# Two routed mixture layers on one core: the last scatters of the convolution phase and the first block weights at other places in the program

## The chip, the cores and the metric

The kernel runs on one NeuronCore of a Trainium2 chip. What counts is the device time of one execution in microseconds (us). PE is the matrix engine (TensorE), DVE VectorE, ACT ScalarE, POOL GpSimd and SP SyncE, which here issues transfers alone. Sixteen DMA engines carry every transfer, whichever queue issues it.

## The reference

`x` has 4 x 3584 tokens of 192 numbers. A causal convolution with 7 taps comes first (one softmaxed kernel for each of 8 groups of 24 columns), then two top-1 mixture layers over its 14336 rows. Cut to what matters:

```
x   = conv(x, softmax(weight))                  # 14336 rows of 192
for layer in (0, 1):
    logits = x @ w_gate                         # 8 experts
    e      = argmax(logits, 1)
    gate   = softmax(logits)[e]                 # in layer 1 also * sigmoid(x @ w_output_gate)[e]
    x[i]   = gate[i] * (relu(x[i] @ w1[e]) @ w2[e])     # w1 192x1024, w2 1024x192
```

## The kernel before

**The convolution phase** has 8 steps of 16 windows of 112 rows. In a step PE convolves, transposes the rows and computes the gate's logits; DVE picks the expert of each row (`step_choose`), and PE's `ranks` and DVE's `step_place` give each row its place in a buffer sorted by expert (`rows[0]` in HBM). POOL then writes the step's rows there with 16 indirect DMAs of 112 rows each (`scatter_step`): 8 of them, then the maximum of the next step's weights, then the other 8. In step 7 no weights follow, so the second half of step 6's scatters stands right behind its first half, and the 16 of step 7 come as soon as their indices are there (`index_ready`).

**The tiles.** Each layer then has 60 tiles, numbered 0 to 59 and 60 to 119, four to a quad. A tile is 256 sorted rows of one expert. PE multiplies them with w1 in four chunks (`hidden`), each of which raises `h_done`; ACT makes the high half of the hidden values when it sees `h_done` (L797, `hh`), DVE the low half (L1352, `hl`), and PE multiplies both with w2 (`contract`): chunk 0 of a tile at the end of that tile, chunks 1 to 3 between the next tile's. ACT writes the result to `y` (L809). From quad 4 of each layer on every third tile of a quad is made of two blocks of 128 rows with an expert each; their weights lie in two slots of their own, slot 2 (the memory of `split`) and slot 3 (the memory of `stage`).

**Who sets the order.** Every engine runs a program of its own, written out by hand. SP's is `loads`: at tile g it waits for `h_done` of tile g, issues the first part (w1, 1 MB) of the weights for tile g+1 if the expert changes, the transposes that bring the rows of tile g+2, and after `y_done` the second part (w2, 0.75 MB). Four tiles of a layer, those with `first`, also load slots 2 and 3, a part each. POOL in layer 0's tiles fetches, scales and stores the next layer's weights and scatters the rows of layer 0's results, four indirect DMAs for two tiles (L626), each held back by `paced` until PE has reached a given chunk. `EARLY` says how many tiles of each layer are planned from a part of the counts: the first 14 tiles of layer 0 use rows of steps 0 to 5 alone. Which expert a tile has stands in a table that DVE writes (`tab` row 0); `tab` row 2 holds the change of expert against two tiles before, since even and odd tiles use slots 0 and 1 in turn. `blk` is the table for blocks, done with `table_ready` 3.

Of the kernel before, what the change touches and what calls it, by code (L numbers as in the profile page):

```python
# [20 lines left out]
E, F = 8, 1024  # L21
N = B * S
P = 128
# [8 lines left out]
G = 16  # L32
STEPS = WINS // G
SPB = STEPS // B
# [11 lines left out]
NT = WHOLE + MIXED  # L46
GT = 2 * NT
EARLY = (14, 12)
QUADS = NT // 4
MIXQ = QUADS - MIXED  # L50
# [24 lines left out]
def build(nc, x, weight, wg0, w10, w20, wg1, wo1, w11, w21, out):  # L75
    f32, f16, i32 = mybir.dt.float32, mybir.dt.float16, mybir.dt.int32
# [11 lines left out]
    with ctx:  # L88
        def sb(name, shape, dt):
            return ctx.enter_context(nc.sbuf_tensor(name, shape, dt))  # L90

        def sem(name):
            return ctx.enter_context(nc.semaphore(name))
# [73 lines left out]
        took = sb("took", [P, E], f32)  # L167
        offr = sb("offr", [P, E + 1], f32)
        start = sb("start", [P, 1], f32)
        ge = sb("ge", [P, NT, E], f32)  # L170
        gt = sb("gt", [P, NT, E], f32)
        te = sb("te", [P, NT], f32)
        tst = sb("tst", [P, NT], f32)
        tew = sb("tew", [P, NT], f32)
        tabD = sb("tabD", [P, GT], f32)
        tab = sb("tab", [P, 3, GT], i32)
# [67 lines left out]
        table_ready = sem("table_ready")  # L244
# [18 lines left out]
        def late(t, n):  # L263

            return not isinstance(t, int) or t >= n
# [9 lines left out]
        def quad(body, i, prep, l, mix):  # L275

            for c in range(4):
                body(i * 4 + c, i * 2 + c // 2, c % 2, c // 2, i, prep, l, mix)

        def layer_of(g, l):  # L280

            return int(g >= NT) if isinstance(g, int) else l
# [46 lines left out]
                 ((QUADS + 2, QUADS + MIXQ, False, False), (QUADS + MIXQ, 2 * QUADS - 1, False, True)))  # L329
        TAIL = range(GT - 4, GT)  # L330
        LAST = (GT - 1, (GT - 1) // 2, 1)
        assert NT % 4 == 0 and 1 < MIXQ < E + 1 < QUADS - 1 and max(EARLY) <= 4 * MIXQ and 12 <= min(EARLY) and STEPS == E and SPB == 2

        def steps(eng, body):

# [38 lines left out]
        def _(sp):  # L374
# [24 lines left out]
            for n in range(STEPS):  # L399
                other = (n + 1) % 2  # L400
# [23 lines left out]
            def load_x(g, x, l):  # L424
                load_rows(tab[0:1, 1, bass.ds(g, 1)], 0, T, x, l, x_loaded[x], meta_loaded[x])
# [5 lines left out]
            def expert(g):  # L431
                return sp.value_load(tab[0:1, 0, bass.ds(g, 1)], min_val=0, max_val=E - 1)

            def block_expert(i, a):
                return sp.value_load(blk[0:1, 0, a, bass.ds(i, 1)], min_val=0, max_val=E - 1)

            def load_w_part(e, l, slot, part):
                cols = (slice(0, W2H), slice(W2H, WCOL))[part]
                sp.dma_start(wslots[slot][:, cols], images[l][bass.ds(e + l, 1), :, cols].rearrange("e p c -> (e p) c")).then_inc(w_loaded[part][slot], 16)

            def change(g):
                return sp.value_load(tab[0:1, 2, bass.ds(g, 1)], min_val=1 - E, max_val=E - 1)
# [13 lines left out]
            def loads(g, k, s, v, i, prep, l, mix):  # L456

                last = g if isinstance(g, int) else 0
                other = isinstance(g, int) and g + 1 in (EARLY[0], EARLY[0] + 1, NT, NT + 1, NT + EARLY[1], NT + EARLY[1] + 1)
                c, ahead = 2 * v + s, layer_of(g + 1, l)  # L460
                first = isinstance(g, int) and i % QUADS == MIXQ - 1
                again = mix and c == 3 and not (isinstance(g, int) and i % QUADS == QUADS - 1)
                needs = []
                if late(g, 1):
                    sp.wait_ge(h_done, g * NP)
                    sp.sem_inc(store_turn, 1)
                    if last + 1 < GT and not (mix and c == 1):
                        needs.append((None if other else change(g + 1), lambda: expert(g + 1), ahead, 1 - s))
                for need in needs:
                    load_next(*need, 0)  # L470
                if last + 2 < GT:
                    if late(g, 1):
                        sp.wait_ge(meta_out, g)
                    if mix and c == 0:
                        load_blocks(i, 2, l)
                    else:
                        load_x(g + 2, (c + 2) % XS, layer_of(g + 2, l))
                if first:
                    load_w_part(block_expert(i + 1, v), l, 2 + v, s)
                for a in range(2 if again else 0):  # L480
                    needs.append((block_change(i + 1, a), lambda a=a: block_expert(i + 1, a), l, 2 + a))
                    load_next(*needs[-1], 0)
                if needs:
                    sp.wait_ge(y_done, g)
                    sp.sem_inc(store_turn, 1)
                for need in needs:
                    load_next(*need, 1)
# [6 lines left out]
            first = [expert(g) for g in range(2)]  # L494
# [9 lines left out]
            for g in HEAD:  # L504
                one(loads, g)
            with sp.Fori(1, 2) as i:
                quad(loads, i, False, 0, False)
            sp.wait_ge(pads_ready, 1)
            for c in range(E // 2):
                one(loads, 8 + c)  # L510
                for e in (2 * c, 2 * c + 1):
                    store_pad(sp, 0, e)
            sp.wait_ge(table_ready, 3)
            for i in range(2 * SLOTS):
                sp.wait_ge(scat_a[i], 8 * G * len(range(i // 2, STEPS, SLOTS)))
            for g in range(12, 4 * MIXQ):
# [19 lines left out]
            sp.wait_ge(table_ready, 5)  # L536
            for v in range(2):
                sp.wait_ge(scat_p[v], 16 * W2T * (PAIRS // 2))
            with sp.Fori(QUADS + 2, QUADS + MIXQ - 1) as i:
                quad(loads, i, False, 1, False)  # L540
            sp.wait_ge(table_ready, 6)
            for g in range(NT + 4 * MIXQ - 4, NT + 4 * MIXQ):
                one(loads, g)
            sp.wait_ge(pads_stored, 32 * E)
            with sp.Fori(QUADS + MIXQ, 2 * QUADS - 1) as i:
# [6 lines left out]
        def _(pool):  # L552
# [37 lines left out]
            def step(n, b, q):  # L590
                if late(n, 1):
                    scatter_step(n - 1, 0, G // 2)
                if n + 1 < STEPS:
                    weight_maxima(n + 1, 1 - q)
                if late(n, 1):
                    scatter_step(n - 1, G // 2, G)

            def weight_maxima(j, slot):
# [4 lines left out]
            def scatter_step(n, w0, w1):  # L603
                if w0 == 0:
                    pool.wait_ge(index_ready, n + 1)
                    pool.sem_inc(pool_turn, 1)
                for w in range(w0, w1):
                    nc.gpsimd.indirect_dma_start(  # L608
                        rows[0][:, :], bass.IndirectOffsetOnAxis(idxa[0:WIN, n % SLOTS, w:w + 1], 0),
                        rowa[n % SLOTS][0:WIN, w, :], None, bounds_check=ROWS - 1,  # L610
                        oob_is_err=False).then_inc(scat_a[2 * (n % SLOTS) + w // (G // 2)], 16)

            weight_maxima(0, 0)
            steps(pool, step)
            scatter_step(STEPS - 1, 0, G)
            def paced(chunk):
                pool.wait_ge(h_done, chunk)
                pool.sem_inc(pool_turn, 1)

            def scatter_row(p, v, j):  # L620
                if j == 0:
# [433 lines left out]
        def _(dve):  # L1055
            V = nc.vector
# [236 lines left out]
            def table_tiles(l, g0, n, unit, first, whole):  # L1293

                at_ = tidx[:, g0:g0 + n] if unit == T else bidx[:, 0:n]
                b3 = lambda a: a.unsqueeze(2).broadcast_to((P, n, E))
                e3 = lambda a: a.unsqueeze(1).broadcast_to((P, n, E))
                link(V.tensor_tensor(ge[:, 0:n, :], b3(at_), e3(cum[:, :]), ALU.is_ge))
                link(V.tensor_tensor(gt[:, 0:n, :], ge[:, 0:n, :], e3(til[:, :]), ALU.mult))
                V.tensor_reduce(tst[:, 0:n], gt[:, 0:n, :], AX.X, ALU.add)  # L1300
                link(V.tensor_reduce(te[:, 0:n], ge[:, 0:n, :], AX.X, ALU.add))
                link(V.scalar_tensor_tensor(tst[:, 0:n], at_, float(unit), tst[:, 0:n], ALU.mult, ALU.add))
                row = row_of(l, g0, n, unit)
                if first:
                    V.tensor_scalar(row, entries(tst, n, unit), float(CAP * E), None, ALU.min)
                else:
                    V.tensor_scalar(row, entries(tst, n, unit), start[:, 0:1], float(CAP * E), ALU.add, ALU.min)
                link(V.tensor_scalar(tew[:, 0:n], te[:, 0:n], float(E - 1), None, ALU.min))
                if unit == T:
                    V.tensor_tensor(tab[:, 2, g0 + 2:g0 + n], tew[:, 2:n], tew[:, 0:n - 2], ALU.subtract)  # L1310
                else:
                    te2 = entries(tew, n, unit)
                    V.tensor_tensor(blk[:, 2, :, g0 + 1:g0 + MIXED], te2[:, :, 1:MIXED], te2[:, :, 0:MIXED - 1], ALU.subtract)
                V.tensor_copy(expert_of(l, g0, n, unit), entries(tew, n, unit)).then_inc(table_ready, 1)
# [221 lines left out]
```

## Time and profile before

| | |
|---|---|
| median of 3 runs | 1329.62 us (1328.49 to 1333.94) |
| the profiled execution | 1330.72 us |
| its span, first to last instruction | 1329.2 us |
| PE busy | 1175.1 us, 88% of the span |
| DVE / ACT / POOL busy | 855.4 / 615.7 / 438.4 us |
| mean granted PE clock | 0.926 of full |

The profile has the start, length and engine of each instruction, and for each wait the engine or DMA that ended it. Where no instruction's end explains the update that ended a wait, the row says "remote"; where an engine waited for nothing that the profile shows, it says "issue". The convolution phase takes the first 250 us or so, the tiles the rest.

### The profile page before, as it was taken

How to read it: one execution, taken by the hardware profiler on the slowest of the kernel's cores; microseconds unless marked ns; L12 is line 12 of the kernel's file. 1: busy time of each engine (PE TensorE's matmuls, PEld its weight loads, DVE VectorE, ACT ScalarE, POOL GpSimd, SP SyncE). 2: the span in 40 equal slices, each digit the busy share in tenths (PEclk: the TensorE clock that was granted, in tenths of full speed). 3: DMA queues.
4: the chain of work that ended last, by engine and by line, in shares of the span. 5: the costliest groups of instructions: out<-in, count | busy, mean ns of one | idle time of the engine just before them, and what ended most of it. 6: DMA issues, size and time to landing. Idle time of an engine off the chain costs nothing.

```text
span 1329.2 us, 38842 instructions
## 1 busy us (share of the span) xinstructions
PE 1175.1 (88%) x13470; PEld 1063.7 (80%) x13470; DVE 855.4 (64%) x2331; ACT 615.7 (46%) x1083; POOL 438.4 (33%) x478
## 2 busy tenths in 40 slices
PE   3767565379998999999999999999999999999996
PEld 2666564358886888888999989788899998999996
DVE  3888778448996998998777787654333433434332
ACT  2766666125554555555555444333333333333332
POOL 1277767522432433333222222322222222222222
PEclk9676765679998999999999999999999999999998
DMA  8677864728979789856544446338824545424451
GB/s 253 193 228 252 255 212 141 210 46 207 231 219 313 144 232 293 231 156 192 140 105 103 106 104 160 64 105 197 247 58 111 163 114 162 114 53 105 113 135 52
DMA packets 236335, 216.61 MB, mean 163 GB/s; under 512 B 176927, under 2 KB 209339, under 8 KB 230114
## 3 DMA queue, kind: packets, MB, share of 16 engines
q1 hardware_dynamic: 209696, 150.68, 43.3%
q0 software_dynamic: 25520, 64.49, 16.2%
q8 instruction: 41, 0.67, 0.2%
q10 hardware_dynamic: 1042, 0.47, 0.2%
q14 instruction: 36, 0.29, 0.1%
HBM read 116.05 MB, written 69.62 MB: 140 GB/s over the span
## 4 chain that ended last, share of the span: by engine, by line
PE 60%; DVE 19%; issue 8%; DMA 4%; another core or an unknown queue 3%; ACT 3%; SPq 2%; DVEq 0%; POOL 0%; ACTq 0%; POOLq 0%
PE bank L856 59%; DMA wslot<-image 2%; DVE am L1120 2%; DVE hl L1352 2%; DVE split L1195 1%; PE bank L861 1%; DVE wam L1084 1%; DVE split L1198 1%; ACT rowt L713 1%; DVE wslot L1222 1%; DVE rowab L1129 1%; DVE rowt L1129 1%; DMA stage<-in_moe_w 1%; DVE wam L1082 1%
## 5 line engine op out<-in xcount | busy, mean ns | idle before, releaser
L1352 DVE SCALAR_TENSOR_TENSOR hl<-bank,hh 128x512 f16<-128x512 f32 x480 | 331.1, 690 | 360.8 <-ACT hh L797 319.3
L797 ACT ACTIVATE hh<-bank 128x512 f16<-128x512 f32 x480 | 286.2, 597 | 487.7 <-PE bank L856 403.5
L856 PE MATMUL bank<-xT,wslot 128*128 128x256 f16 (+1 forms) x3920 | 468.0, 275 | 15.1 <-issue 7.2
L856 PE MATMUL bank<-wslot,hh 128*128 128x192 f16 x3136 | 425.8, 248 | 12.8 <-DMA wslot<-image 6.6
L856 PE MATMUL bank<-wslot,hl 128*128 128x192 f16 x1568 | 388.5, 248 | 2.0 <-issue 2.0
L856 PEld LDWEIGHTS bank<-xT,wslot 128*128 128x128 f16 (+1 forms) x3920 | 328.7, 98 | 74.0 <-issue 31.1
L856 PEld LDWEIGHTS bank<-wslot,hh 128*128 128x128 f16 x3136 | 281.0, 98 | 34.1 <-issue 24.6
L685 POOL DMA_INDIRECT out_tokens<-y,idxt x120 | 117.1, 976 | 365.6 <-ACT y L809 311.9
L626 POOL DMA_INDIRECT rows<-rowt,idxp x120 | 126.3, 1053 | 328.0 <-PE bank L856 194.3
L856 PEld LDWEIGHTS bank<-wslot,hl 128*128 128x128 f16 x1568 | 154.5, 99 | 2.1 <-issue 1.8
L608 POOL DMA_INDIRECT rows<-rowab,idxa x96 | 108.0, 1125 | 64.1 <-issue 43.5
L856 PE MATMUL bank<-xw,band 128*112 128x192 f32 x256 | 73.8, 469 | 53.2 <-ACT conv L713 24.7
L713 ACT ACTIVATE rT<-bank 128x672 f16<-128x672 f16 (+1 forms) x124 | 95.3, 772 | 54.1 <-PE bank L861 47.1
L856 PEld LDWEIGHTS bank<-xw,band 128*112 128x112 f32 x256 | 66.9, 272 | 56.3 <-ACT conv L713 23.8
L809 ACT ACTIVATE y<-bank,tf 128x192 f32<-128x192 f32 x240 | 87.9, 417 | 48.4 <-PE bank L856 47.8
L856 PE MATMUL bank<-xT,split 128*128 128x128 f16 (+1 forms) x880 | 102.0, 220 | 0.4 <-issue 0.2
L856 PE MATMUL bank<-xT,stage 128*128 128x128 f16 (+1 forms) x880 | 102.0, 220 | 0.0
L856 PEld LDWEIGHTS bank<-xT,split 128*128 128x128 f16 (+1 forms) x880 | 77.0, 98 | 3.9 <-issue 1.3
L856 PEld LDWEIGHTS bank<-xT,stage 128*128 128x128 f16 (+1 forms) x880 | 77.9, 98 | 0.3 <-issue 0.2
L856 PEld LDWEIGHTS bank<-gs,rT 128*112 128x112 f16 (+1 forms) x744 | 47.6, 142 | 31.3 <-ACT rT L713 24.9
L856 PE MATMUL bank<-gs,rT 128*112 128x16 f16 (+1 forms) x744 | 54.7, 202 | 19.8 <-ACT rT L713 19.2
L856 PE MATMUL bank<-split,hh 128*128 128x192 f16 x352 | 58.1, 247 | 0.0
(173 smaller groups left out, 1275.6 us busy)
## 6 DMA issues: line engine op xcount, KB each, us to landing
wslot<-image SPq DMA_DIRECT2D x22, 1024.0 KB
wslot<-image SPq DMA_DIRECT2D x22, 768.0 KB
split<-image SPq DMA_DIRECT2D x16, 1024.0 KB
split<-image SPq DMA_DIRECT2D x16, 768.0 KB
image<-split POOLq DMA_DIRECT2D x18, 512.0 KB
image<-split SPq DMA_DIRECT2D x8, 1024.0 KB
image<-split POOLq DMA_DIRECT2D x9, 768.0 KB
stage<-in_moe_w SPq DMA_DIRECT2D x8, 768.0 KB
```

Of the source, the lines that this page charges most:

```text
L608: nc.gpsimd.indirect_dma_start(rows[0][:, :], bass.IndirectOffsetOnAxis(idxa[0:WIN, n % SLOTS, w:w + 1], 0), rowa[n % SLOTS][0:WIN, w, :], ...
L626: nc.gpsimd.indirect_dma_start(rows[1][:, :], bass.IndirectOffsetOnAxis(idxp[:, v, j:j + 1], 0), rowt[:, v, j, :], None, bounds_check=ROWS ...
L685: nc.gpsimd.indirect_dma_start(out[:, :], bass.IndirectOffsetOnAxis(idxt[:, s, j:j + 1], 0), y[:, s, j, :], None, bounds_check=N - 1, oob_ ...
L713: return nc.scalar.activation(o, i, ACT.Copy)
L797: nc.scalar.activation(hh[:, c, :], bank[c][:, :], ACT.Relu).then_inc(hh_out, 1)
L809: last = nc.scalar.activation(y[:, s, j, :], bank[YB + s][:, j * D:(j + 1) * D], ACT.Identity, scale=tf[:, s, j:j + 1])
L856: return nc.tensor.matmul(o, a, b_, start=start, stop=stop, skip_group_check=True)
L861: last = nc.tensor.transpose(dst(c), src[:, c * P:(c + 1) * P], ident[0:src.shape[0], 0:src.shape[0]])
L1082: V.tensor_reduce(wam[:, slot, 0:1], stage[:, slot, 0:2 * F], AX.X, ALU.max, apply_absolute_value=True)
L1120: link(V.tensor_reduce(am[0:nrows, 0:nwins], src, AX.X, ALU.max, apply_absolute_value=True))
L1129: return V.tensor_tensor(row[:, :, D + DB:2 * D], scaled[:, :, 0:P], row[:, :, 0:P], ALU.subtract)
L1352: V.scalar_tensor_tensor(hl[:, c, :], bank[c][:, :], 0.0, hh[:, c, :], ALU.max, ALU.subtract).then_inc(hl_out, 1)
```

## The change

Three things. On POOL the second half of step 6's scatters and all 16 of step 7's are issued one by one, scatter c when PE has done chunk c * 2 // 3 + 1 of the tiles (`h_done`), which spreads the 24 over the 16 chunks of tiles 0 to 3. On SP the four `first` tiles of each layer are tiles 8 to 11 instead of 12 to 15 (and 68 to 71 instead of 72 to 75), and the wait for the block table stands ahead of tile 8. On DVE two more columns of the table of changes are filled in (`last2`), so that tiles 14, 15, 72 and 73 load weights only if the expert changes, where they always did.

```
-                if late(n, 1):
+                if 1 <= n < STEPS - 1:
                     scatter_step(n - 1, G // 2, G)
...
             steps(pool, step)
-            scatter_step(STEPS - 1, 0, G)
+
             def paced(chunk):
                 pool.wait_ge(h_done, chunk)
                 pool.sem_inc(pool_turn, 1)
+
+            for c in range(3 * G // 2):
+                paced(c * 2 // 3 + 1)
+                if c < G // 2:
+                    scatter_step(STEPS - 2, G // 2 + c, G // 2 + c + 1)
+                else:
+                    scatter_step(STEPS - 1, c - G // 2, c - G // 2 + 1)
...
-                other = isinstance(g, int) and g + 1 in (EARLY[0], EARLY[0] + 1, NT, NT + 1, NT + EARLY[1], NT + EARLY[1] + 1)
+                other = isinstance(g, int) and NT <= g + 1 < NT + 2
...
-                first = isinstance(g, int) and i % QUADS == MIXQ - 1
+                first = isinstance(g, int) and i % QUADS == MIXQ - 2
...
                 if first:
-                    load_w_part(block_expert(i + 1, v), l, 2 + v, s)
+                    load_w_part(block_expert(i + 2, v), l, 2 + v, s)
...
             sp.wait_ge(pads_ready, 1)
+            sp.wait_ge(table_ready, 3)
             for c in range(E // 2):
                 one(loads, 8 + c)
                 for e in (2 * c, 2 * c + 1):
                     store_pad(sp, 0, e)
-            sp.wait_ge(table_ready, 3)
...
-            with sp.Fori(QUADS + 2, QUADS + MIXQ - 1) as i:
-                quad(loads, i, False, 1, False)
             sp.wait_ge(table_ready, 6)
-            for g in range(NT + 4 * MIXQ - 4, NT + 4 * MIXQ):
+            for g in range(NT + 4 * MIXQ - 8, NT + 4 * MIXQ):
                 one(loads, g)
...
                     V.tensor_tensor(tab[:, 2, g0 + 2:g0 + n], tew[:, 2:n], tew[:, 0:n - 2], ALU.subtract)
+                    if not first:
+                        V.tensor_tensor(tab[:, 2, g0:g0 + 2], tew[:, 0:2], last2[:, :], ALU.subtract)
+                    else:
+                        V.tensor_copy(last2[:, :], tew[:, n - 2:n])
```

On POOL, at the end of the convolution phase, the program of before has these rows (`rowab` and `idxa` hold a step's rows and places; the first eight are step 6's first half):

```order
L608 DMA rows<-rowab,idxa 116992x194 [waits index_ready]
L608 DMA rows<-rowab,idxa 116992x194 x15
L608 DMA rows<-rowab,idxa 116992x194 [waits index_ready]
L608 DMA rows<-rowab,idxa 116992x194 x15
L657 UNCONDITIONAL_BRANCH
```

At the same place of the changed program stand:

```order
L607 DMA rows<-rowab,idxa 116992x194 [waits index_ready]
L607 DMA rows<-rowab,idxa 116992x194 x7
L607 DMA rows<-rowab,idxa 116992x194 [waits h_done] x8
L607 DMA rows<-rowab,idxa 116992x194 [waits h_done,index_ready]
L607 DMA rows<-rowab,idxa 116992x194 [waits h_done] x15
L663 UNCONDITIONAL_BRANCH
```

So 24 of the 32 scatters now wait for PE's chunks; nothing was put between them, and the loop over the next layer's weights still follows them.

On SP, at tile 8, behind the rows for tile 10 (`xT`, `xmeta`), the program of before goes straight to the wait for `y_done` and the second part of the next tile's weights (`wslot`):

```order
L420 DMA_TRANSPOSE xT<-rows 128x3x256
L421 ISA
L421 DMA_TRANSPOSE xT<-rows 128x1x256
L422 ISA
L422 DMA xmeta<-rows 128x2x2
L451 COMPARE_AND_BRANCH [waits y_done]
L432 TENSOR_LOAD tab
L432 ISA x2
L439 ISA
L439 DMA wslot<-image 128x3072
```

In the changed program the first part of slot 2 (`split`) stands between them:

```order
L421 DMA_TRANSPOSE xT<-rows 128x3x256
L422 ISA
L422 DMA_TRANSPOSE xT<-rows 128x1x256
L423 ISA
L423 DMA xmeta<-rows 128x2x2
L436 TENSOR_LOAD blk
L436 ISA x2
L440 ISA
L440 DMA split<-image 128x4096
L452 COMPARE_AND_BRANCH [waits y_done]
L433 TENSOR_LOAD tab
L433 ISA x2
```

What moved there is one load of a register and one 1 MB transfer, from tile 12 to tile 8; tiles 9, 10 and 11 get theirs likewise, and two stores of padding rows (`padrow`) follow at each of these tiles in both programs.

## Rows read from the trace of the kernel before

**Rows 1.** The page's slices, 40 of 33.2 us each, in tenths
```profile
PE   3767565379998999999999999999999999999996
DMA  8677864728979789856544446338824545424451
```

**Rows 2.** Windows: length, busy us (count) by engine, PE clock, DMA share, GB/s
```profile
236.00:252.00 16.00, 1.83 (x24) 1.75 (x25) 2.60 (x9) 1.04 (x2) 7.58 (x9) 0.50 0.75 191
252.00:280.00 28.00, 13.80 (x92) 9.29 (x89) 13.99 (x56) 2.98 (x5) 15.37 (x16) 0.68 0.48 136
```

**Rows 3.** Timeline, end of the convolution phase: start, length, engine, line; [idle before]
```profile
236.34 0.94 POOL L608 DMA_INDIRECT rows<-rowab,idxa  x1 [0.30 <-issue]
...
238.49 0.73 ACT L713 ACTIVATE rT<-bank 128x672 f16<-128x672 f16 x1 [4.35 <-remote]
...
239.28 0.72 PE L856 MATMUL bank<-gs,rT 128*112 128x16 f16 x6 [4.36 <-ACT rT L713]
...
245.08 0.94 POOL L608 DMA_INDIRECT rows<-rowab,idxa  x1 [0.30 <-issue]
...
248.79 0.42 DVE L1137 TENSOR_REDUCE lg<-bank 112x128 f32<-112x256 f32 x1 [13.72 <-remote]
```

**Rows 4.** Timelines of PE, ACT, DVE and POOL during tile 0
```profile
251.97 5.79 PE L856 MATMUL bank<-xT,wslot 128*128 128x256 f16 x40
...
264.44 1.88 PE L856 MATMUL bank<-xT,wslot 128*128 128x256 f16 x12
...
260.71 0.60 ACT L797 ACTIVATE hh<-bank 128x512 f16<-128x512 f32 x1 [4.07 <-remote]
271.40 0.60 ACT L797 ACTIVATE hh<-bank 128x512 f16<-128x512 f32 x1 [10.09 <-remote]
277.94 0.60 ACT L797 ACTIVATE hh<-bank 128x512 f16<-128x512 f32 x1 [5.94 <-remote]
...
261.73 1.88 DVE L1352 SCALAR_TENSOR_TENSOR hl<-bank,hh 128x512 f16<-128x512 f32 x3
...
273.69 0.94 POOL L608 DMA_INDIRECT rows<-rowab,idxa  x1 [0.30 <-issue]
```

**Rows 5.** Timeline, last scatter of a convolution step and what follows
```profile
164.96 0.94 POOL L608 DMA_INDIRECT rows<-rowab,idxa  x1 [0.30 <-issue]
...
167.77 0.29 DVE L1175 TENSOR_TENSOR posm<-bank,base 112x128 f32<-112x128 f32 x1 [4.37 <-remote]
```

**Rows 6.** Waits in 300 to 800 us: total us, times, longest
```profile
ACT hh L797 <- PE bank L856: 138.9, 136, 8.4
```

**Rows 7.** DMA queues, 262 to 280 and 280 to 300 us: packets, MB, share
```profile
q0 software_dynamic: 530, 0.96, 17.9%
...
q8 instruction: 1, 0.02, 0.3%
...
rows<-rowab,idxa POOLq DMA_INDIRECT x11
...
q8 instruction: 1, 0.02, 0.5%
```

**Rows 8.** Timeline of ACT: results of tiles 7, 11 and 15
```profile
346.89 0.73 ACT L809 ACTIVATE y<-bank,tf 128x192 f32<-128x192 f32 x2 [0.25 <-PE bank L856]
...
383.11 0.73 ACT L809 ACTIVATE y<-bank,tf 128x192 f32<-128x192 f32 x2 [0.25 <-PE bank L856]
...
429.23 0.73 ACT L809 ACTIVATE y<-bank,tf 128x192 f32<-128x192 f32 x2 [0.25 <-PE bank L856]
```

**Rows 9.** A wait in 376 to 430 us, and transfers of 384 to 424 us
```profile
PE bank L856 <- DMA wslot<-image: 7.8, 3, 4.2
...
DMA packets 6716, 13.87 MB, mean 347 GB/s; under 512 B 4497, under 2 KB 4609, under 8 KB 6075
```

**Rows 10.** Windows around tiles 8 to 11 and tiles 71 to 75
```profile
340.00:380.00 40.00, 39.13 (x461) 34.06 (x459) 37.63 (x103) 22.05 (x36) 15.71 (x17) 1.00 0.75 197
...
900.00:940.00 40.00, 39.57 (x430) 35.43 (x428) 15.57 (x35) 15.16 (x30) 9.02 (x10) 1.00 0.89 234
```

More of the change, by code:

```diff
@@ L169, in build @@
         start = sb("start", [P, 1], f32)
+        last2 = sb("last2", [P, 2], f32)
         ge = sb("ge", [P, NT, E], f32)
@@ L331, in build @@
         LAST = (GT - 1, (GT - 1) // 2, 1)
-        assert NT % 4 == 0 and 1 < MIXQ < E + 1 < QUADS - 1 and max(EARLY) <= 4 * MIXQ and 12 <= min(EARLY) and STEPS == E and SPB == 2
+        assert NT % 4 == 0 and MIXQ == 4 and MIXQ < E + 1 < QUADS - 1 and max(EARLY) <= 4 * MIXQ and 12 <= min(EARLY) and STEPS == E and SPB == 2
         def steps(eng, body):
```

## The prediction

> **What bounds the kernel now.** I read the page's slices first: PE is busy nine tenths or more of nearly every slice from the tenth on [rows 1]. The chain of the tiles is PE's, so a change pays only where PE stands. Two holes stand out: the slice from 232 to 266 us (PE 3) and the one from 399 to 432 us (PE 8). DMA is high in both, at 7 and 8 [rows 1], so each could be a matter of bytes. I took them apart by windows and timelines.
>
> The first hole. From 236 to 252 us PE is busy 1.83 us, from 252 to 280 us 13.80 of 28 us, at a granted clock of 0.50 and 0.68, that is mostly on the lower of its two levels, 1.2 GHz [rows 2]. The timeline shows a strange thing. PE's last logits end at 240.00, DVE, which waits for them alone, goes on at 248.79, and its row says "remote": no instruction's end explains the update [rows 3]. Before it ACT waited 4.35 us for transposes in the same way. It goes on in tile 0: all 40 matmuls of its four chunks are on record by 257.76, but ACT sees the third chunk at 260.71 and the fourth at 271.40; the first chunk of tile 1 ends at 266.32 and ACT sees it at 277.94 [rows 4]. So PE's signals reach the others 3 to 12 us late. Meanwhile POOL issues scatters without a pause, eight from 236.34 to 246.02, one each 1.25 us, and the sixteen of step 7 in the same way until 274.63; both times the late signal comes 2.8 and 3.3 us after the last of them [rows 3, 4]. In the convolution steps the same: the last scatter ends at 165.90, DVE goes on at 167.77 [rows 5]. In tiles whose scatters are paced, 300 to 800 us, the waits name no remote releaser at all; ACT waits for PE's own records, 1.0 us in the mean (138.9 us over 136) [rows 6]. I read this as: a long unbroken run of scatters holds up PE's signals. I can't see by what.
>
> The second hole is a plain one. Tiles 7 to 11 take 36.22 us, tiles 11 to 15 take 46.12 us [rows 8], 9.9 us more. PE waits 7.8 us there for weights, and the DMA engines move 13.87 MB in 40 us, 347 GB/s, nothing left free [rows 9].
>
> **The change, part by part.** (a) Eight scatters of step 6 leave the stretch from 236 to 246 us. The first eight stay and end at about 236, so I leave ACT's late copy at 238.49 as it is. PE's logits then end at 240.0, and DVE goes on at 240.1 instead of 248.79: 8.7 us. (b) The sixteen of step 7 no longer run in one piece through tile 0. In the trace DVE needs 12.94 us from its restart to the low half of chunk 0 (248.79 to 261.73, choosing, placing and the tables), and PE 4.59 us more to the end of tile 1's first chunk (261.73 to 266.32) [rows 3, 4]. With DVE at 240.1 that chunk ends at 257.6, and without a late signal ACT takes it there and not at 277.94: 20.3 us for (a) and (b) together. What could hold it: PE may start tile 0 only when its rows and weights are there. Their issue by SP is not moved, and the engines are 0.75 busy up to 252 us [rows 2]; tile 1's weights are issued behind them and could land after PE asks. I bound that by nothing and by 5 us and take 1.5.
>
> (c) The price of the spread: the 24 scatters still go out, within 16 chunks of about 2.26 us (tiles 7 to 11 take 36.22 us for 16 chunks [rows 8]). That is one each 1.5 us, hardly thinner than 1.25 us in the run. But now POOL waits for the very signal that a run delays: at most two go out, then it stands until the next chunk is seen. Bounds: nothing, if short groups do no harm, as in the tiles from 300 us on [rows 6], and 2.95 us a chunk, the least lateness of tile 0's third chunk (257.76 to 260.71) [rows 4], which is 47 us over 16 chunks. The nearest rows are those of the paced tiles, so I take 2 us in all. POOL's fetch of the next layer's weights stands behind the last scatter, which now waits for chunk 16, as the fetch did anyway: it starts 1.25 us later, and PE does not wait for it in tiles 4 and 5; if that cover were gone, it would cost these 1.25 us.
>
> The trace gives a scatter's share of the DMA engines: software queue 17.9% of 18 us for 11 scatters, 0.29 us each [rows 7], so the eight that leave (a) free 2.3 us of traffic. The Trainium skill, in "Trainium Kernel Development and Optimization", section Key Constraints, says that DMAs from SP, ACT and POOL run on the same 16 engines and interleave, and that issuing from several queues saves issue time only. By that rule a scatter costs its traffic wherever it stands, and (a) and (b) would give 2 us; by the rows above they give 17. I go by the rows, since the engines are only 0.48 busy while the signals are latest [rows 2]; the rule's way is a rival below.
>
> (d) Block weights: 3.67 MB (four parts, 1 + 0.75 MB twice) leave the stretch of 384 to 424 us. At 347 GB/s [rows 9] they occupy it for 10.6 us, a little over what tiles 11 to 15 lose. Not all of it returns: two tiles change expert in this stretch anyway, and part of the blocks' bytes lies behind the transfer that PE waits for. I take 8 of the 9.9 us, bounds 3 and 9.9. In tiles 8 to 11 the engines are 0.75 busy over 40 us [rows 10], so 10 us are free for 10.6 us of load; SP's rows for tile g+2 queue behind it but have a tile of slack. I charge 1 us, bounds 0 and 4. In layer 1 tiles 71 to 75 have PE busy 39.57 of 40 us at a DMA share of 0.89 [rows 10]: no hole to fill, nothing.
>
> (e) The conditional loads of tiles 14, 15, 72 and 73. Even and odd tiles walk through the experts in order, from an early plan and then from the rest, where both start anew; so the expert changes at 14 and 15 in all likelihood, and the transfers stay. At nothing. If both fell away, another 3.67 MB would go from the same stretch, but then the hole is closed already. (f) Four small DVE operations, some 0.2 us each, and the wait for the block table, which DVE has written by tile 1: nothing.
>
> Sum: 20.3 - 1.5 - 2 + 8 - 1 = 23.8 us. The profiled execution took 1330.7 us, of which 1329.2 are its span, so 1306.9; the median of the runs is 1.1 us less: **1306 us**. A measurement of this kernel tells 0.5%, 6.6 us, from no change.
>
> **The rivals.**
> 1. *The signals are late for another reason.* All engines enter new code at that point, and traffic is dense there. For: 236 to 262 us is both. Against: the signals are latest from 262 to 278 us, at low traffic, and a fetch of instructions was seen once there, as in the 20 us after it, where nothing stood [rows 7]. Then only the traffic of (a), 2 us, and (d) minus its charge, 7 us, come: 1322 us. The page "Runtime: NRT & Kernel Launch", section Instruction fetch mechanics, of the Trainium skill says that code is refilled in blocks of 16 KiB by DMA and that a jump out of the loaded window stalls. By that rule the stand would stay where it is. Chance 0.13, with the shared-engines rule's way, which gives the same time.
> 2. *Half a gain.* Either the run of the first eight scatters suffices to hold DVE, or tile 0 waits for its rows and weights, or pairs of scatters cost 0.5 us a chunk (8 us): 10 to 16 us in all, 1314 to 1320 us. Chance 0.2.
> 3. *Slower: the spread keeps every chunk late.* One mechanism: each of the 16 chunks of tiles 0 to 3 carries one or two scatters and its signal comes late. For: 1.5 us apart is near 1.25 us. Against: the paced tiles [rows 6]. At the 2.95 us of the third chunk it is 47 us against the other terms' 25.8: 1330 + 21 = 1351 us. It decides from 1.6 us a chunk on (25.8 us over 16), which is no change. Chance 0.05 for slower, 0.06 for a price between 1.2 and 2 us a chunk, which ends within 0.5%.
>
> **How the numbers follow.** Forecast 0.56 (1299 to 1313 us: full gain of both parts 1299.5; 17 us 1313). Rival 1 straddles the bound of 6.6 us (1323): I count 0.07 of it as same. So faster 0.82, same 0.13, slower 0.05. The range reaches over rival 2 and most of rival 1: 1297 to 1322 us.
>
> **What would show it.** DVE's `lg` within 1 us of PE's last logits; no remote waits of ACT's `hh` over 1 us in tiles 0 to 3; tile 1's first chunk near 257 us, the result of tile 7 near 330 instead of 346.89; tiles 11 to 15 in 36 to 39 us. If the late signals stay with the scatters apart, my reading of the first hole is wrong; if tiles 8 to 11 get longer by what 11 to 15 lose, (d) is.

## The result, and the profile after

The changed kernel takes 1318.28 us in the median of 4 runs (1317.81 to 1319.69), the kernel before on the same chip 1329.35 us (4 runs): a ratio of 0.9916, interval 0.9898 to 0.9935. It is faster by 11.1 us where I had forecast 23.6, less than half; the time lies inside the range of 1297 to 1322 us that I gave. The profiled execution took 1318.32 us, its span 1316.8 us.

Windows of the changed kernel, columns as in [rows 2]: the first hole, and tiles 9 to 11.

```profile
236.00:252.00 16.00, 9.27 (x75) 6.84 (x74) 11.05 (x50) 2.97 (x5) 4.16 (x5) 0.52 0.84 226
252.00:280.00 28.00, 23.41 (x233) 19.99 (x231) 17.33 (x57) 7.80 (x15) 15.40 (x17) 0.94 0.58 145
340.00:380.00 40.00, 32.96 (x364) 29.04 (x363) 30.34 (x87) 19.03 (x32) 9.50 (x13) 0.91 0.99 239
```

In the first two PE is busy 32.7 us, where it was 15.6 [rows 2], and from 252 us on the granted clock is 0.94, near the upper level of 2.4 GHz. The third answers to the first of [rows 10]: PE had 39.13 us there and has 32.96, DMA went from 0.75 to 0.99. So one hole is mostly filled, and there is a new one.

The timeline at the end of the convolution phase shows how the first hole filled.

```profile
238.04 0.95 POOL L607 DMA_INDIRECT rows<-rowab,idxa  x1 [0.30 <-issue]
240.06 0.73 ACT L719 ACTIVATE rT<-bank 128x672 f16<-128x672 f16 x1 [2.27 <-remote]
240.85 0.72 PE L862 MATMUL bank<-gs,rT 128*112 128x16 f16 x6 [2.28 <-ACT rT L719]
241.68 0.42 DVE L1143 TENSOR_REDUCE lg<-bank 112x128 f32<-112x256 f32 x1 [3.35 <-PE bank L862]
```

While the first eight scatters go out, ACT still waits for a remote releaser and goes on 2.0 us behind the start of the last of them. The second eight are gone, and DVE's `lg` follows PE's logits at once, where it had waited 13.72 us [rows 3]. One pattern is the same in both kernels, in a convolution step that the change doesn't touch:

```profile
167.84 0.94 POOL L607 DMA_INDIRECT rows<-rowab,idxa  x1 [0.30 <-issue]
170.67 0.29 DVE L1181 TENSOR_TENSOR posm<-bank,base 112x128 f32<-112x128 f32 x1 [4.39 <-remote]
```

`posm` starts 2.83 us behind the start of the last scatter of its run, as it did before (2.81 us, [rows 5]). Both times there are 2.9 us between the kernels: the changed one was already 2.7 us behind at the first `posm` (61.08 and 58.35 us), before any instruction that was edited.

ACT's timeline gives the results of tiles 0 to 3, 7, 9, 10, 11 and 15 in the changed kernel; the last three are to be read against [rows 8].

```profile
264.59 0.73 ACT L815 ACTIVATE y<-bank,tf 128x192 f32<-128x192 f32 x2
275.11 0.73 ACT L815 ACTIVATE y<-bank,tf 128x192 f32<-128x192 f32 x2 [0.39 <-PE bank L862]
286.76 0.73 ACT L815 ACTIVATE y<-bank,tf 128x192 f32<-128x192 f32 x2 [3.75 <-remote]
297.00 0.73 ACT L815 ACTIVATE y<-bank,tf 128x192 f32<-128x192 f32 x2 [0.47 <-PE bank L862]
...
333.27 0.73 ACT L815 ACTIVATE y<-bank,tf 128x192 f32<-128x192 f32 x2 [0.25 <-PE bank L862]
...
350.94 0.73 ACT L815 ACTIVATE y<-bank,tf 128x192 f32<-128x192 f32 x2 [0.25 <-PE bank L862]
365.27 0.73 ACT L815 ACTIVATE y<-bank,tf 128x192 f32<-128x192 f32 x2
377.69 0.73 ACT L815 ACTIVATE y<-bank,tf 128x192 f32<-128x192 f32 x2 [0.47 <-PE bank L862]
...
415.62 0.73 ACT L815 ACTIVATE y<-bank,tf 128x192 f32<-128x192 f32 x2 [0.25 <-PE bank L862]
```

In the kernel before these results stand at 284.47, 292.88, 300.99 and 310.14 us for tiles 0 to 3. So tile 0 is 19.9 us earlier, tile 3 only 13.1: the spread costs 6.8 us in tiles 1 to 3. Tile 7 is 13.6 us earlier. Tiles 8 to 11 take 44.42 us and had taken 36.22; tiles 12 to 15 take 37.93 us and had taken 46.12. At tile 15 it is again 13.6 us, and at the last tile (1308.81 us, before 1321.28) 12.5.

Where the 6.8 us go is seen best in tile 2 of the changed kernel (11.65 us, before 8.11), in the timeline of POOL, ACT and PE.

```profile
280.28 0.94 POOL L607 DMA_INDIRECT rows<-rowab,idxa  x1 [1.86 <-PE bank L862]
...
285.39 0.94 POOL L607 DMA_INDIRECT rows<-rowab,idxa  x1 [0.30 <-issue]
286.76 0.73 ACT L815 ACTIVATE y<-bank,tf 128x192 f32<-128x192 f32 x2 [3.75 <-remote]
...
288.40 0.53 PE L867 MATMUL bank<-ident,rowt 128*128 128x128 f16 x6 [2.36 <-ACT rT L719]
288.75 2.86 PE L862 MATMUL bank<-xT,wslot 128*128 128x256 f16 x16
```

POOL does not send one or two scatters and then stand. It had fallen behind its paces and sent five in a row here, 1.25 to 1.36 us apart; of the 24 scatters 21 go out in groups of three or five. ACT waited 3.75 us for a remote releaser and wrote `y` only 1.4 us behind the start of the fifth, PE stood 2.36 us behind ACT, and its next 16 matmuls took 2.86 us where the same 16 had taken 1.58 us (303.32 us in the kernel before); the granted clock is 0.56 from 288.4 to 291.6 us. In tile 0 a group of five (249.91 to 254.92 us) has ACT's `hh` wait 2.92 us for a remote releaser. In tile 1 the rows name PE, and only the times show a late signal: PE's third chunk ends at 262.09 us and ACT takes it at 264.10, behind a group of three.

The new hole is in tile 10. The chain of waits, and then the waits of 340 to 380 us (total, times, longest):

```profile
349.37 12.70 DMA image<-split
...
365.42 0.61 DVE rowt L1135
366.16 0.82 PE bank L867 x6
```

```profile
ACT split L741 <- DMA image<-split: 5.9, 1, 5.9
PE bank L867 <- DVE rowt L1135: 7.0, 2, 6.8
DVE hl L1362 <- ACT hh L803: 7.8, 4, 6.1
```

POOL stores 768 KB of the next layer's weight image at 349.37. ACT writes the next half into the same buffer (`split`), so it has to wait until the store has landed, and in its queue that write stands between the first and the second `hh` of a tile. With the moved block weights beside it (a 1 MB part was issued at 353.72 us) the store took 12.70 us; ACT stood 5.9, DVE and PE behind ACT. In the kernel before the same store and the same write of ACT are these:

```profile
362.99 0.57 POOL L654 DMA_DIRECT2D image<-split  x1
...
368.42 1.57 ACT L735 ACTIVATE split<-stage,winv 128x1536 f16<-128x1536 f32 x1
```

There the write starts 5.4 us behind the store's issue and waits for nothing, so the store needed at most that.

### The profile page after: what moved, and what is told of

It is laid out like the page before. It is cut to its first block, busy times and chain, and to the rows that moved or that the text cites. A ratio compares the mean times of both kernels' runs of the same rounds, so it can differ in the third digit from the quotient of the medians.

```text
span 1316.8 us, 38885 instructions
## 1 busy us (share of the span) xinstructions
PE 1172.9 (89%) x13470; PEld 1061.8 (81%) x13470; DVE 856.1 (65%) x2335; ACT 616.1 (47%) x1083; POOL 439.7 (33%) x478
## 4 chain that ended last, share of the span: by engine, by line
PE 59%; DVE 15%; issue 9%; DMA 5%; ACT 4%; SPq 3%; another core or an unknown queue 2%; POOL 2%; DVEq 0%; POOLq 0%; ACTq 0%
PE bank L862 58%; DVE am L1126 2%; DVE hl L1362 2%; DMA wslot<-image 2%; DMA image<-split 2%; POOL rows L607 1%; PE bank L867 1%; DVE split L1201 1%; DVE wam L1090 1%; ACT rowt L719 1%; DVE wslot L1228 1%; SPq L421 1%; DVE rowt L1135 1%; DMA stage<-in_moe_w 1%
## 5 line engine op out<-in xcount | busy, mean ns | idle before, releaser
L862 PE MATMUL bank<-xT,wslot 128*128 128x256 f16 (+1 forms) x3920 | 468.5, 275 | 11.0 <-DVE hl L1362 5.3
L862 PE MATMUL bank<-wslot,hh 128*128 128x192 f16 x3136 | 423.4, 247 | 6.2 <-issue 3.2
L862 PE MATMUL bank<-wslot,hl 128*128 128x192 f16 x1568 | 387.1, 247 | 0.5 <-issue 0.5
L862 PEld LDWEIGHTS bank<-xT,wslot 128*128 128x128 f16 (+1 forms) x3920 | 329.1, 98 | 69.6 <-issue 23.2
L862 PEld LDWEIGHTS bank<-wslot,hh 128*128 128x128 f16 x3136 | 280.0, 98 | 26.4 <-issue 17.3
L862 PEld LDWEIGHTS bank<-wslot,hl 128*128 128x128 f16 x1568 | 154.0, 98 | 1.7 <-issue 1.6
L862 PE MATMUL bank<-xw,band 128*112 128x192 f32 x256 | 72.8, 465 | 55.1 <-ACT conv L719 24.4
L862 PEld LDWEIGHTS bank<-xw,band 128*112 128x112 f32 x256 | 66.2, 269 | 58.2 <-ACT conv L719 23.5
L862 PE MATMUL bank<-xT,split 128*128 128x128 f16 (+1 forms) x880 | 100.9, 219 | 0.7 <-issue 0.4
L862 PE MATMUL bank<-xT,stage 128*128 128x128 f16 (+1 forms) x880 | 100.9, 218 | 0.0
L862 PEld LDWEIGHTS bank<-xT,split 128*128 128x128 f16 (+1 forms) x880 | 76.4, 97 | 3.8 <-issue 1.1
L862 PEld LDWEIGHTS bank<-xT,stage 128*128 128x128 f16 (+1 forms) x880 | 77.4, 97 | 0.6 <-issue 0.5
L862 PEld LDWEIGHTS bank<-gs,rT 128*112 128x112 f16 (+1 forms) x744 | 48.6, 145 | 29.9 <-ACT rT L719 22.6
L862 PE MATMUL bank<-gs,rT 128*112 128x16 f16 (+1 forms) x744 | 55.5, 204 | 18.7 <-ACT rT L719 17.3
L862 PE MATMUL bank<-split,hh 128*128 128x192 f16 x352 | 58.0, 247 | 0.0
```

What stands on the lines that cost most here:

```text
L862: return nc.tensor.matmul(o, a, b_, start=start, stop=stop, skip_group_check=True)
```

## The experiments

They ran on a second chip, and that became the main finding. The kernel before takes **1279.81 us** there (29 runs, 1275.07 to 1285.2), 50 us less than on the first. That it is a chip and not a state of one is an inference from these times: the four runs on the first lie at 1328 to 1334 us, and nothing lies between. Each ratio below is against the kernel before on the second chip; the times in the expectations were written for the first. The changed kernel as a whole was not measured on the second chip.

**The scatters alone.** The kernel before with POOL's part of the change:

```diff
-                if late(n, 1):
+                if 1 <= n < STEPS - 1:
                     scatter_step(n - 1, G // 2, G)
...
-            scatter_step(STEPS - 1, 0, G)
+            for c in range(3 * G // 2):
+                paced(c * 2 // 3 + 1)
...
```

> Only the scatters are spread over the chunks of tiles 0 to 3; block weights and SP as before. Theory (the two parts are separate, the spread gave 13 us by tile 3 and the moved block weights nothing net): tile 3's result 13 us sooner than before, tiles 11 to 15 still about 46 us, in all about 1317 us, as the whole change. Rival (the block weights' move gave part of the gain, and something in tiles 4 to 15 took it away again): 1310 us if the move cost, 1323 us if it paid.

1282.56 us (12 runs), ratio 1.0021, interval 1.0002 to 1.0041: nothing gained, and by this interval a little lost. The trace has no remote wait at all from 200 to 300 us, and the result of tile 0 stands at 239.11 us. Tiles 1, 2 and 3 take 8.46, 8.11 and 9.15 us; so here the spread cost them nothing. One thing is late, in ACT's results of tiles 4 and 5 and in the chain of waits:

```profile
272.98 0.73 ACT L815 ACTIVATE y<-bank,tf 128x192 f32<-128x192 f32 x2 [0.39 <-PE bank L862]
287.86 0.73 ACT L815 ACTIVATE y<-bank,tf 128x192 f32<-128x192 f32 x2
```

```profile
267.87 14.82 DMA stage<-in_moe_w
282.71 0.06 DVE wam L1090
```

The fetch of the next layer's weights is what the forecast called covered. Its first part goes out 4.0 us ahead of tile 3's result (260.88 and 264.83 us), where it goes out 7.1 us ahead in the next experiment: 3.2 us later, not the 1.25 us of the forecast. Its last part needed 14.82 us to land, DVE waited for it, and tile 5 took 14.88 us instead of the 9.50 of the next experiment.

**The block weights alone.** The changed kernel with POOL's part undone:

```diff
-                first = isinstance(g, int) and i % QUADS == MIXQ - 1
+                first = isinstance(g, int) and i % QUADS == MIXQ - 2
...
-                    load_w_part(block_expert(i + 1, v), l, 2 + v, s)
+                    load_w_part(block_expert(i + 2, v), l, 2 + v, s)
```

> Only the block weights are loaded four tiles sooner, with the wider table of changes; scatters as before. Theory (what tiles 12 to 15 gain, tiles 8 to 11 lose): 1328 to 1331 us, tiles 7 to 11 about 44 us and tiles 11 to 15 about 38 us. Rival (the stand in tiles 8 to 11 comes only with the scatters spread): tiles 7 to 11 stay at 36 us, 1321 us.

1281.63 us (12 runs), ratio 1.0021, interval 1.0000 to 1.0043. Nothing gained either. ACT's results of tiles 7, 11 and 15, and the chain in tile 10:

```profile
304.29 0.73 ACT L809 ACTIVATE y<-bank,tf 128x192 f32<-128x192 f32 x2 [0.25 <-PE bank L856]
...
346.76 0.73 ACT L809 ACTIVATE y<-bank,tf 128x192 f32<-128x192 f32 x2 [0.47 <-PE bank L856]
...
386.52 0.73 ACT L809 ACTIVATE y<-bank,tf 128x192 f32<-128x192 f32 x2 [0.25 <-PE bank L856]
```

```profile
320.37 11.20 DMA image<-split
```

Tiles 8 to 11 take 42.47 us and tiles 12 to 15 39.76. With the scatters alone, whose block weights stand where they did, it is 35.87 and 46.23 us. So the edit takes 6.5 us from one stretch and puts 6.6 into the other, and the same store, 11.20 us long, is in the chain. The theory held and the rival did not: the stand in tiles 8 to 11 comes with the scatters left alone.

This trace has the scatters where the kernel before has them, sixteen in one piece across tile 0, and it too has no remote wait. Its tile 0 is late for another reason. The waits of 200 to 300 us for tile 0's rows, here and with the scatters alone:

```profile
PE bank L856 <- DMA xT<-rows: 7.8, 1, 7.8
PE bank L862 <- DMA xT<-rows: 4.4, 1, 4.4
```

From step 7's `posm` to tile 0's result it is 21.75 us (220.98 to 242.73) here and 19.56 (219.55 to 239.11) with the scatters spread. So on this chip the spread did give tile 0 something, 2.2 us, by the wait for its rows, and tile 5 took it back.

**All 24 scatters in one run, after the first chunk.** If a run holds up the signals, this has the longest one of all, 30 us, right across tiles 0 to 3.

```diff
+            paced(1)
+            scatter_step(STEPS - 2, G // 2, G)
+            scatter_step(STEPS - 1, 0, G)
```

> The 24 scatters go out in one unbroken run from tile 0's first chunk on; everything else as before. Theory (an unbroken run holds up PE's signals until it ends, and the pacing breaks it): remote waits of ACT's hh of 5 to 12 us during the run's 30 us, tile 1's result 10 us or more later than with the spread, in all about 1325 to 1330 us. Rival (only the place matters, not the pacing): within 2 us of the spread alone, about 1317 us.

1277.98 us (10 runs), ratio 0.9992, interval 0.9975 to 1.0009. The window of that run, columns as in [rows 2]:

```profile
226.00:256.00 30.00, 28.90 (x302) 25.38 (x300) 21.23 (x63) 12.14 (x23) 22.80 (x24) 0.97 0.73 168
```

POOL has its 24 scatters there, 22.80 us of them in 30, and PE is busy 28.90 us at a granted clock of 0.97. The timeline inside it:

```profile
227.43 0.94 POOL L608 DMA_INDIRECT rows<-rowab,idxa  x1 [0.30 <-issue]
...
227.57 0.60 ACT L800 ACTIVATE hh<-bank 128x512 f16<-128x512 f32 x1 [1.58 <-PE bank L859]
228.66 0.60 ACT L800 ACTIVATE hh<-bank 128x512 f16<-128x512 f32 x1 [0.50 <-PE bank L859]
228.68 0.94 POOL L608 DMA_INDIRECT rows<-rowab,idxa  x1 [0.30 <-issue]
229.54 0.60 ACT L800 ACTIVATE hh<-bank 128x512 f16<-128x512 f32 x1 [0.28 <-PE bank L859]
229.92 0.94 POOL L608 DMA_INDIRECT rows<-rowab,idxa  x1 [0.30 <-issue]
```

ACT takes three chunks while scatters go out at the same 1.25 us, and no wait of the whole trace has a remote releaser. Tile 1's result comes 8.42 us behind tile 0's, as with the spread. The theory failed on this chip, and the rival stands. And the untouched convolution step, beside the pair from the changed kernel above:

```profile
150.72 0.94 POOL L608 DMA_INDIRECT rows<-rowab,idxa  x1 [0.30 <-issue]
...
151.16 0.70 PE L859 MATMUL bank<-oh,ones 112*128 112x128 f16 x16
151.96 0.94 POOL L608 DMA_INDIRECT rows<-rowab,idxa  x1 [0.30 <-issue]
152.80 0.28 DVE L1178 TENSOR_TENSOR posm<-bank,base 112x128 f32<-112x128 f32 x1
153.21 0.94 POOL L608 DMA_INDIRECT rows<-rowab,idxa  x1 [0.30 <-issue]
```

`posm` starts in the midst of the run, 0.9 us behind the end of PE's matmuls. On this chip a run holds up no signal.

**All 24 in one run, after chunk 16.** The same with `paced(16)`; one run, with its profile.

> The 24 scatters go out in one unbroken run, but only once PE has done chunk 16, the last of tile 3. Theory (the scatters hold up PE's signals): in tiles 0 to 3 no wait of ACT's hh for a remote releaser, tile 0's result at about 264 us or sooner and tiles 1 to 3 at 8.5 us each, while remote waits appear in tiles 4 to 7 during the run. Rival (new code or dense traffic holds up the signals): tile 0's remote waits stay at 10 us or more, and none appear in tiles 4 to 7. The next layer's weights start some 30 us later here, so its total says little.

1296.8 us. Tiles 0 to 3 are those of the others (239.45 us, then 8.41, 8.11 and 9.15), so once tile 0 has its rows the scatters' traffic costs these tiles nothing. No remote wait appears anywhere, so this run can't tell the theory from its rival. The window after them:

```profile
280.00:300.00 20.00, 0.00 (x0) 0.00 (x0) 2.42 (x2) 0.00 (x0) 12.76 (x16) 0.50 0.67 159
```

PE does nothing for 20 us and tile 5 takes 34.18 us: POOL's fetch of the next weights stands behind 24 scatters, and everything waits for it. This is the price of a scatter in POOL's queue when the cover is gone, and it is the fetch, not the scatter, that has to be watched.

## Why the prediction was right and wrong

**The first hole, (a) and (b): right in place, size and pattern, on the first chip alone.** I expected tile 0 to gain 20.3 - 1.5 = 18.8 us and it gained 19.9, or 22.8 when counted from the late start of 2.9 us. The 1.5 us for tile 0's rows came as 1.6 (`PE bank L862 <- DMA xT<-rows`, 200 to 300 us). `lg` follows PE's logits, as forecast. One sign failed: no remote wait of `hh` over 1 us was to be left in tiles 0 to 3, and one of 2.92 us was. That the run of scatters is what is waited for has, on that chip, the pattern of [rows 5] in both traces, and the end of the wait where the run was cut. No experiment was made there; and on the second chip a run of 24 held up no signal, nor did the sixteen of the kernel before; what they cost there is the 2.2 us by which tile 0's rows come late. So "a long unbroken run of scatters holds up PE's signals" is no rule of this kernel. It describes what the traces of one chip show.

**The price of the spread, (c): the first mis-sized term.** I took 2 us of a range of 0 to 47, "at most two go out, then it stands". It cost 6.8 us in tiles 1 to 3. The step that failed is that sentence, and with it the bound "short groups do no harm": POOL catches up in groups of three and five, and each group is a short run of the kind that I had just found guilty. [rows 6] end at 800 us. Further on, in tiles whose scatters go out in pairs, the trace of the kernel before has waits of ACT's `hh` for a remote releaser (first line, 960 to 1280 us); at the same stretch of the second chip (24 in one run, 905 to 1225 us) there is none:

```profile
ACT hh L797 <- remote: 31.9, 10, 3.3
ACT hh L800 <- PE bank L859: 179.0, 129, 1.6
```

Each of the ten ends 1.6 to 1.8 us behind the start of the second scatter of a pair. They cost little there, since PE is busy 319.1 of the 320 us, but they say that behind a group of two a signal can be late already. The price of rival 2 (pairs at 0.5 us a chunk, 8 us) is near the measured one, and the gain of 11.1 us lies in its 10 to 16; but it counted on the gain of (d), so the agreement of the time is luck. On the second chip the price in tiles 1 to 3 was 0, and 5.4 us came at tile 5 by the fetch behind the last scatter, which I had put at 1.25 us at the most.

**The block weights, (d): the gain right, the charge wrong by seven.** Tiles 12 to 15 gained 8.2 us (forecast 8), tiles 8 to 11 lost 8.2 (forecast 1, bound 4). All six traces, of two chips, agree: about 36 + 45 to 46 us in the old order, 42 to 44 + 38 to 40 us in the new. The step that failed is the charge. It came from "10 us are free for 10.6 us of load", which counted only PE's own transfers. It left out who else waits for a transfer in that stretch: ACT, for a store of 768 KB, with PE's next chunks behind it in its queue. The chain shows this store in both traces with the moved weights, at 12.70 and 11.20 us against at most 5.4 in the kernel before. That holding back one part until the store has landed, or loading the blocks behind tiles 2 and 3, would win the 8 us back was not measured, and remains an argument from the trace.

The page "Trainium Kernel Development and Optimization" of the Trainium skill, section Key Constraints, says that the DMAs of SP, ACT and POOL run on the same 16 engines and interleave. The trace agrees, at 12.70 us for this store in a stretch with a DMA share of 0.99; in the prediction I had weighed the rule only for the scatters, and did not apply it to the store.

**The sum.** 19.9 - 6.8 = 13.1 us at tile 3, + 0.5 by tile 7, - 8.2 + 8.2 to tile 15, and 1.1 us less by the last tile, which I did not trace to a cause: 12.5, and 11.1 between the medians. With a spread price of 2 and a charge of 1, that is 4.8 and 7.2 us less, it would have been 23.1 us. **(e)** holds: tiles 14 and 15 change their expert and fetch their weights in both kernels. No run shows **(f)** by itself.

**The rivals.** Against rival 1, another reason for the late signals, speaks the first chip: the waits went where the scatters went and did not stay at the place. Its time, 1322 us, was made of 2 us of scatter traffic and (d); on the second chip the 2 us came almost to the number (2.2 at tile 0), with no late signal at all. Rival 3, every chunk late, did not come. What I did not have as a rival is that the largest term is there on one chip and not on the other.

**What stays open.** Why the first chip delays signals beside POOL's scatters and the second doesn't. The scatters themselves look alike in both traces (0.94 us, 1.25 us apart). Of the 50 us between the chips 41.7 are there at tile 0's result, when the two traces with the scatters in their old place are compared (284.47 us, and 242.73 with the block weights alone). From the first `posm` to that of step 6 the first chip takes 162.5 us and the second 140.4, 3.7 us less a step, and the rest is in the stand at the end of the phase.

## What to carry to other kernels

Before an edit is costed on a wait that names no releaser, look whether the same wait exists on another chip: the largest term here, 20 us of a forecast of 24, was 2 us on the second. Look too at the whole trace for such waits and not at one stretch of it: the pairs past 960 us would have told that short groups are not free. When bytes are moved into a stretch that "has room", list every engine that waits for any transfer in it, stores too, and what stands behind that wait in its queue. And a pace that counts finished work does not keep instructions apart: once the queue has fallen behind, they go out in groups.

## What was not expected of the hardware

- The same kernel takes 1329.35 us in the median on one chip and 1279.81 us on another. On the first, `posm` starts 2.8 to 3.0 us behind the start of the last scatter in the second to the sixth convolution step (1.2 us in the seventh); on the second it starts in the midst of them, within 1 us of the end of PE's matmuls.
- A store of 768 KB from SBUF took 12.70 and 11.20 us beside the moved weight parts, and at most 5.4 us without them. The last part of the next weights, 768 KB from POOL's queue, needed 14.82 us at tile 5.
- With PE idle for 20 us the granted clock of the window is 0.50, the lower of its two levels (1.2 GHz); in the run of 24 scatters with PE busy 28.90 of 30 us it is 0.97, near 2.4 GHz.
